# Loading, rounding and subtracting the first four chunks' first matrices by blocks of channels

## The chip, the cores and the metric

The kernel runs on one core of one Trainium2 chip. The metric is the device time of one execution in microseconds (us). Engines are named as in the profile: PE is TensorE (PEld its weight loads), DVE is VectorE, ACT is ScalarE, POOL is GpSimd, SP is SyncE, whose queue issues nearly all DMAs.

## What is computed

The reference, cut to what matters:

```python
# attention: batch 2, 8 heads, 576 positions, head size 64, window of 64 keys
scores = q @ k.T / 8, masked to 0 <= i - j < 64
attn = softmax(scores);  x = attn @ v            # -> x: 1152 tokens x 512
# four experts, all of them on every token
p = domain_probs / domain_probs.sum(-1)
out = sum over e of p[:, e] * (relu(x @ w1[e]) @ w2[e])      # 512 -> 1024 -> 512
# last network
h = out @ w_in;  result = (h * cos(h)) @ w_out   # 512 -> 2048 -> 512
```

Every large product is made of three matmuls in a reduced format: both operands are split into a rounded part (`_hi`) and what rounding left (`_lo`), and hi x hi, hi x lo and lo x hi are added up.

## The kernel before

**Tiling.** The 1152 tokens are three tiles of 384. The attention is cut into 12 units m = 0 to 11, one for each tile and each pair of heads; a unit fills one of the four channel blocks (128 channels each) of x for its tile. Units 0 to 3 (`AHEAD` = 4) give tile 0. The hidden layer of an expert is cut into 8 chunks f of 128 hidden units; a chunk's weights are 128 partitions x 1024 numbers: the first 512 (the chunk's first matrix, for x @ w1) are four blocks of 128 columns, one for each channel block c of x, and the other 512 are the second matrix (for the product with w2).

**Staging of weights.** A chunk comes by DMA into `w_raw` (four slots). ACT or DVE rounds it into `w_hi`. POOL subtracts, `w_lo` = `w_raw` - `w_hi`, in pieces of 256 numbers (L424). Of expert 0's first four chunks (`FIRST` = 4) the two matrices are handled apart: `load_half(f, 0)` loads the first matrix of chunk f (L317), `high_half(f)` rounds it (ACT L589 for f = 0, 1; DVE L846 for f = 2, 3), `low_half(f)` subtracts (L428). `load_half(f, 1)`, `high_second(f)` and `low_second(f)` (L435) do the same for the second matrix. Chunk 4 comes whole into a spare buffer inside `h_raw` (L341) and is treated by `high_ahead` and `low_ahead` (L598, L439). Chunks 5, 6 and 7 are loaded by `load_later` (L321) into slots 0, 1, 2 of `w_raw`: it waits until `low_second(slot)` has read the slot for the last time.

**The attention of a unit.** PE `scores(m)` (L1109); DVE `masked_maxima(m, h)` (L816) for both heads h; ACT `exponentials(m, h)` (L568); DVE `invert_sums(m, h)` (L829); POOL `normalise(m, h)` (L447, the line of its instruction is L450); PE `transpose_probs(m, h)` (L1127, instruction L1142); DVE copies of the transposed rows, `copy_first` (L836) and `copy_second_early` (L841), from unit 4 on ACT `copy_second` (L579); PE `outputs(m)` (L1145); ACT `x_high(m)` (L585); DVE `x_low(m)` (L850).

**The first product runs under the attention.** As soon as unit m has filled channel block m of x, PE runs `up_ahead(m, fs)` (L1170): the products of block m for the chunks fs, three matmuls (L1166) for each chunk. So c = 0 uses only the first block of 128 columns of each first matrix, c = 1 the second one, and so on. Only for c = 0 does `up_ahead` wait for weights, chunk by chunk (L1173, L1174).

**Order.** Each engine's order is written out by hand. PE's is at L1352 to L1415, POOL's at L455 to L481, ACT's at L720 to L763, DVE's at L1010 to L1069, SP's at L327 to L362. Each engine and each queue works strictly in its written order; a wait at one instruction holds all that stands behind it.

Of the kernel before, what the change touches and what calls it, by code (L numbers as in the profile page):

```python
# [108 lines left out]
def build(nc, q, k, v, probs, weights, out):  # L109
    with ExitStack() as ctx:  # L110
# [3 lines left out]
        def sem(name):  # L114
            return ctx.enter_context(nc.semaphore(name))
# [98 lines left out]
        x_hi_done = sem("x_hi_done")  # L214
        x_lo_done = sem("x_lo_done")
        dp_in, dp_done, p_picked = sem("dp_in"), sem("dp_done"), sem("p_picked")
        half_in = [sem(f"half_in{i}") for i in range(FIRST)]
        w_in_done = [sem(f"w_in_done{i}") for i in range(STAGE)]
        second_in = [sem(f"second_in{i}") for i in range(FIRST)]
        ahead_in = sem("ahead_in")  # L220
        half_hi_done = sem("half_hi_done")
        half_hi_done_dve = sem("half_hi_done_dve")
        half_lo_done = sem("half_lo_done")
        second_hi_done = sem("second_hi_done")
        second_lo_done = sem("second_lo_done")
        w_hi_done = sem("w_hi_done")
# [68 lines left out]
        def _(sp):  # L295
            def load_qk(m):
                t, c, r = m // PAIRS, m % PAIRS, m % SLOTS
                if m >= SLOTS:
                    sp.wait_ge(scored, m - SLOTS + 1)
                sp.dma_start(q_t[:, r, :], q[c, :, t * TOK:(t + 1) * TOK]).then_inc(q_in[r], 16)  # L300
                n = TOK if t == 0 else KEYS
                sp.dma_start(k_t[:, r, 0:n], k[c, :, KEY0[t]:KEY0[t] + n]).then_inc(k_in[r], 16)

            def load_v(m):
                t, c, r = m // PAIRS, m % PAIRS, m % SLOTS
                if m >= SLOTS:
# [7 lines left out]
                sp.wait_ge(w_lo_done, n - STAGE + 1)  # L314
                sp.dma_start(w_raw[:, f % STAGE, :], weights[e, f]).then_inc(w_in_done[f % STAGE], 16)

            def load_half(f, half, landed):  # L317
                cols = slice(half * DM, (half + 1) * DM)
                sp.dma_start(w_raw[:, f, cols], weights[0, f, :, cols]).then_inc(landed[f], 16)

            def load_later(f):  # L321

                slot = f - FIRST - 1
                sp.wait_ge(second_lo_done, slot + 1)
                sp.dma_start(w_raw[:, slot, :], weights[0, f]).then_inc(w_in_done[slot], 16)

# [2 lines left out]
            load_qk(1)  # L329
            load_qk(2)  # L330
            load_v(0)
            for f in range(FIRST):
                load_half(f, 0, half_in)
            load_qk(3)
            load_v(1)
            load_qk(4)
            load_v(2)
            load_half(0, 1, second_in)
            load_qk(5)
            load_v(3)  # L340
            sp.dma_start(w_ahead, weights[0, FIRST]).then_inc(ahead_in, 16)  # L341
            load_half(1, 1, second_in)
            load_qk(6)
            load_half(2, 1, second_in)
            load_v(4)
            load_later(5)
            load_half(3, 1, second_in)
            load_qk(7)
            load_v(5)
            load_qk(8)  # L350
# [7 lines left out]
            load_qk(11)  # L358
            for e in range(1, E):
                load_v(8 + e)  # L360
            sp.wait_ge(second_lo_done, FIRST)
            sp.wait_ge(w_lo_done, FC)  # L362
            def load_block(e, f):
# [24 lines left out]
        def _(pool):  # L388
# [32 lines left out]
            def low_part(f, raw, begin, end, part):  # L421

                for at in range(begin, end, part):
                    last = nc.gpsimd.tensor_tensor(w_lo[:, f, at:at + part], raw[:, at - begin:at - begin + part],  # L424
                                                   w_hi[:, f, at:at + part], ALU.subtract)
                return last

            def low_half(f):  # L428
                if f < FIRST // 2:
                    pool.wait_ge(half_hi_done, f + 1)  # L430
                else:
                    pool.wait_ge(half_hi_done_dve, f - FIRST // 2 + 1)
                low_part(f, w_raw[:, f, 0:DM], 0, DM, PART).then_inc(half_lo_done, 1)

            def low_second(f):  # L435
                pool.wait_ge(second_hi_done, f + 1)
                low_part(f, w_raw[:, f, DM:2 * DM], DM, 2 * DM, PART).then_inc(second_lo_done, 1)
# [18 lines left out]
            normalise(0, 1)  # L456
            nc.gpsimd.memset(half_pi[:, :], 0.0).then_inc(half_pi_zeroed, 1)
            normalise(1, 0)
            low_half(0)
            normalise(1, 1)  # L460
            low_half(1)
            low_half(2)
            low_half(3)
            normalise(2, 0)
            normalise(2, 1)
            normalise(3, 0)
            low_second(0)
            normalise(3, 1)
            normalise(4, 0)
            low_ahead(FIRST, w_ahead)  # L470
            normalise(4, 1)
# [89 lines left out]
        def _(act):  # L561
# [24 lines left out]
                act.wait_ge(attended, m + 1)  # L586
                nc.scalar.activation(x_hi[x_cell(m)], o_bank(m)[:, 0:TOK], ACT.Copy).then_inc(x_hi_done, 1)

            def high_half(f):  # L589
                act.wait_ge(half_in[f], 16)  # L590
                nc.scalar.activation(w_hi[:, f, 0:DM], w_raw[:, f, 0:DM], ACT.Copy).then_inc(half_hi_done, 1)

            def high_second(f):
                act.wait_ge(second_in[f], 16)
# [125 lines left out]
            exponentials(0, 0)  # L720
            exponentials(0, 1)
            exponentials(1, 0)
            high_half(0)
            exponentials(1, 1)
            high_half(1)
            for m in range(AHEAD):
                if m > 0:
                    exponentials(m + 2, 0)
# [71 lines left out]
        def _(dve):  # L800
# [42 lines left out]
                nc.vector.tensor_copy(prob_t[:, 1, :, :], pt_bank(m, 1)[:, 0:TOK].rearrange(  # L843
                    "p (t c) -> p t c", t=CT)).then_inc(second_copied_early, 1)

            def high_half(f):  # L846
                dve.wait_ge(half_in[f], 16)
                nc.vector.tensor_copy(w_hi[:, f, 0:DM], w_raw[:, f, 0:DM]).then_inc(half_hi_done_dve, 1)
# [173 lines left out]
            copy_second_early(0)  # L1022
            masked_maxima(2, 1)
            invert_sums(1, 1)
            high_half(2)
            x_low(0)
            high_half(3)
            copy_first(1)
            copy_second_early(1)
            masked_maxima(3, 0)  # L1030
# [4 lines left out]
            for m in range(2, AHEAD):  # L1035
                invert_sums(m + 1, 0)
                masked_maxima(m + 2, 0)
                copy_first(m)
                masked_maxima(m + 2, 1)
                copy_second_early(m)  # L1040
                invert_sums(m + 1, 1)
                x_low(m)
            masked_maxima(AHEAD + 2, 0)
            masked_maxima(AHEAD + 2, 1)
# [59 lines left out]
        def _(pe):  # L1104
# [64 lines left out]

            def up_ahead(c, fs):  # L1170

                for f in fs:
                    if c == 0:  # L1173
                        pe.wait_ge(half_lo_done, f + 1)  # L1174
                    last = up_cells(y_ps[f], f, 0, (c,))
                    if c == DC - 1:
                        last.then_inc(up_done, 1)
# [301 lines left out]
```

## Time and profile before

| | us |
|---|---|
| median of 3 runs | 640.38 (640.38 to 641.29) |
| profiled execution, its own time | 639.62 |
| its span in the trace | 637.7 |
| PE busy | 629.2 (99% of the span) |
| DVE, ACT, POOL busy | 305.2, 260.3, 272.2 |

The 1.92 us between span and own time lie around the program. The profile page gives the busy time of each engine, the chain of work that ended last, and the costliest groups of instructions; a query of the trace gives the instructions in order of time, with the idle time in front of each and the one that ended it. Times in the trace count from the span's start.

### The profile page before, as it was taken

The page shows a single profiled execution, that of the slowest core. Times are in us where ns is not written, and L with a number is a line of the kernel's source. Part 1 is how long each engine was busy: PE and PEld are TensorE (multiplying, and loading weights), DVE is VectorE, ACT ScalarE, POOL GpSimd, SP SyncE. Part 2 cuts the span into 40 slices and gives each one's busy share as a digit, 9 for nine tenths or more (in the row PEclk, how much of TensorE's full clock was granted, in tenths as well). Part 3 has the DMA queues.
Part 4 walks back from the last instruction along what each step waited for, and adds up shares of the span by engine and source line. Part 5 has one row for each costly group of instructions (what it writes and reads, how often), then busy time and mean ns, then how long its engine had stood idle before and what let it go on. Part 6 is the DMA issues. An engine that isn't in the chain of part 4 may idle for free.

```text
span 637.7 us, 10145 instructions
## 1 busy us (share of the span) xinstructions
PE 629.2 (99%) x3656; PEld 561.9 (88%) x3656; DVE 305.2 (48%) x722; ACT 260.3 (41%) x554; POOL 272.2 (43%) x404
## 2 busy tenths in 40 slices
PE   7999999999999999999999999999999999999998
PEld 5887899999989998989998888989999999999996
DVE  6754431215433315433315433426775666766564
ACT  6776322233321223321223321246655467544542
POOL 6783246698720296720296720287000059400000
PEclk9999999999999999999999999999999999999999
DMA  9874100022120011220012120033100012001011
GB/s 285 273 226 151 44 1 1 1 56 77 67 66 1 1 66 66 66 66 0 1 66 67 67 66 1 26 107 100 34 0 1 1 38 96 1 0 49 0 51 50
DMA packets 21896, 37.25 MB, mean 58 GB/s; under 512 B 2784, under 2 KB 14048, under 8 KB 21856
## 3 DMA queue, kind: packets, MB, share of 16 engines
q1 hardware_dynamic: 20688, 36.71, 17.7%
q8 instruction: 24, 0.39, 0.2%
q10 hardware_dynamic: 1168, 0.02, 0.1%
q14 instruction: 16, 0.13, 0.1%
HBM read 34.36 MB, written 2.36 MB: 58 GB/s over the span
## 4 chain that ended last, share of the span: by engine, by line
PE 96%; DVE 1%; POOL 1%; ACT 1%; issue 0%; DVEq 0%
PE bank L1166 31%; PE bank L1194 31%; PE bank L1225 16%; PE bank L1211 14%; PE bank L1158 2%; PE bank L1122 1%; PE bank L1142 1%; PE bank L1308 1%; DVE s_sb L823 1%; PE bank L1350 1%; POOL w_lo L424 0%; ACT prob L574 0%; DVE acc L973 0%; POOL prob L450 0%; DVE prob_t L838 0%
## 5 line engine op out<-in xcount | busy, mean ns | idle before, releaser
L424 POOL TENSOR_TENSOR w_lo<-w_raw,w_hi 128x128 fp32r<-128x128 f32 (+1 forms) x252 | 150.6, 633 | 214.4 <-ACT w_hi L606 211.9
L1166 PE MATMUL bank<-x_hi,w_hi 128*128 128x384 f32 (+1 forms) x384 | 131.2, 342 | 0.5 <-POOL w_lo L424 0.5
L1166 PE MATMUL bank<-x_hi,w_lo 128*128 128x384 f32 (+1 forms) x384 | 129.1, 336 | 0.0
L1166 PE MATMUL bank<-x_lo,w_hi 128*128 128x384 f32 (+1 forms) x384 | 128.7, 335 | 0.0
L1194 PE MATMUL bank<-w_hi,hp_hi 128*128 128x512 f32 x288 | 114.7, 398 | 0.1
L1194 PE MATMUL bank<-w_hi,hp_lo 128*128 128x512 f32 x288 | 113.4, 394 | 0.0
L1194 PE MATMUL bank<-w_lo,hp_hi 128*128 128x512 f32 x288 | 112.1, 389 | 0.0
L926 DVE TENSOR_TENSOR h_raw<-bank,h_raw 128x384 f32<-128x384 f32 x84 | 46.6, 555 | 91.9 <-PE bank L1211 91.9
L1166 PEld LDWEIGHTS bank<-x_hi,w_hi 128*128 128x128 f32 x384 | 72.1, 188 | 3.6 <-POOL w_lo L424 0.8
L1166 PEld LDWEIGHTS bank<-x_lo,w_hi 128*128 128x128 f32 x384 | 72.2, 188 | 1.5
L857 DVE SCALAR_TENSOR_TENSOR hp_lo<-bank,hp_hi 128x384 fp32r<-128x384 f32 x48 | 26.5, 556 | 98.1 <-ACT hp_hi L638 57.5
L1166 PEld LDWEIGHTS bank<-x_hi,w_lo 128*128 128x128 f32 x384 | 72.1, 188 | 0.0
L1194 PEld LDWEIGHTS bank<-w_lo,hp_hi 128*128 128x128 f32 x288 | 54.1, 188 | 12.2
L630 ACT ACTIVATE hp_hi<-h_raw 128x384 fp32r<-128x384 f32 x48 | 25.3, 528 | 94.2 <-DVE h_raw L926 94.2
L1194 PEld LDWEIGHTS bank<-w_hi,hp_hi 128*128 128x128 f32 x288 | 54.0, 188 | 10.9 <-issue 0.4
L1194 PEld LDWEIGHTS bank<-w_hi,hp_lo 128*128 128x128 f32 x288 | 54.2, 188 | 8.5
L1225 PE MATMUL bank<-w_hi,hp_hi 128*128 128x512 f32 x144 | 56.6, 393 | 0.0
L1225 PE MATMUL bank<-w_hi,hp_lo 128*128 128x512 f32 x144 | 56.5, 392 | 0.0
L1225 PE MATMUL bank<-w_lo,hp_hi 128*128 128x512 f32 x144 | 56.1, 390 | 0.0
L606 ACT ACTIVATE w_hi<-w_raw 128x1024 fp32r<-128x1024 f32 x40 | 42.1, 1052 | 11.7 <-PE bank L1194 11.7
L992 DVE TENSOR_TENSOR h_raw<-c_cos,bank 128x384 f32<-128x384 f32 x48 | 26.6, 554 | 37.1 <-ACT c_cos L701 37.1
L699 ACT ACTIVATE c_abs<-c_r 128x384 f32<-128x384 f32 x48 | 25.3, 527 | 42.5 <-DVE c_r L984 42.4
(103 smaller groups left out, 966.4 us busy)
## 6 DMA issues: line engine op xcount, KB each, us to landing
w_raw<-in_weights SPq DMA_DIRECT2D x43, 512.0 KB, 3.7
q_t<-in_q SPq DMA_DIRECT2D x12, 192.0 KB, 4.3
result<-acc SPq DMA_DIRECT2D x9, 256.0 KB, 2.0
w_raw<-in_weights SPq DMA_DIRECT2D x8, 256.0 KB, 5.8
k_t<-in_k SPq DMA_DIRECT2D x8, 224.0 KB, 5.3
v_w<-in_v SPq DMA_DIRECT2D x4, 384.0 KB, 5.0
v_w<-in_v SPq DMA_DIRECT2D x4, 320.0 KB, 6.5
k_t<-in_k SPq DMA_DIRECT2D x4, 192.0 KB, 3.7
```

The costliest lines, as they stand in the source:

```text
L424: last = nc.gpsimd.tensor_tensor(w_lo[:, f, at:at + part], raw[:, at - begin:at - begin + part], w_hi[:, f, at:at + part], ALU.subtract)
L606: nc.scalar.activation(w_hi[:, f, :], w_raw[:, f % STAGE, :], ACT.Copy).then_inc(w_hi_done, 1)
L630: nc.scalar.activation(hp_hi[:, i, :], h_raw[:, i, :], ACT.Relu).then_inc(pair_hi_done, 1)
L699: nc.scalar.activation(c_abs, c_r2, ACT.Abs).then_inc(cos_abs, 1)
L857: nc.vector.scalar_tensor_tensor(out=hp_lo[:, f % HP, :], in0=ps[:, 0:TOK], scalar=0.0, in1=hp_hi[:, f % HP, :], op0=ALU.max, op1=ALU.subt ...
L926: nc.vector.tensor_tensor(h_raw[:, place, :], ps, h_raw[:, other, :], ALU.add).then_inc(pair_taken, 1)
L992: nc.vector.tensor_tensor(h_raw[:, f % HP, :], c_cos, bank_h, ALU.mult).then_inc(cos_taken, 1)
L1158: last = nc.tensor.matmul(o_bank(m)[heads, block_of * WIN:(block_of + 1) * WIN], v_w[:, r, WINDOW_OF[t][block_of], heads], prob_t[:, h, bl ...
L1166: last = nc.tensor.matmul(ps[:, 0:TOK], w[:, f, chunk(c)], x[:, c, token_cols(t)], start=c == 0 and i == 0, stop=c == DC - 1 and i == 2)
L1194: last = nc.tensor.matmul(y_ps[c][:, :], h[:, f % HP, chunk(c)], w[:, f, DM:2 * DM], start=f == 0 and i == 0, stop=f == FC - 1 and i == 2)
L1211: last = nc.tensor.matmul(bank[(g * PRODUCTS + j) % 2][:, 0:TOK], a, b, start=c == 0 and i == 0, stop=c == 1 and i == 2)
L1225: last = nc.tensor.matmul(pair_y[t][c][:, :], h[:, i, chunk(c)], w[:, f, DM:2 * DM], start=f == 0 and k == 0, stop=f == FC - 1 and k == 2)
```

## The change

The first matrices of chunks 0 to 3 are no longer handled chunk by chunk but block by block. `load_channels(c)` loads channel block c of all four chunks in one DMA of the same 256 KB (runs of 128 numbers, 512 bytes, where a half had runs of 2 KB). `high_channels(c)` rounds it, ACT for c = 0, 1 and DVE for c = 2, 3. `low_channels(c)` subtracts it, as two instructions of 2 x 128 numbers. `up_ahead(c, fs)` waits for block c. The five orders change with it.

```diff
+            def load_channels(c):
+                sp.dma_start(w_raw[:, :, chunk(c)],
+                             weights[0, 0:FIRST, :, chunk(c)].rearrange("f p n -> p f n")).then_inc(channels_in[c], 16)
...
             def load_later(f):
                 slot = f - FIRST - 1
+                sp.wait_ge(channels_lo_done, DC)
                 sp.wait_ge(second_lo_done, slot + 1)
...
-            def low_half(f):
-                if f < FIRST // 2:
-                    pool.wait_ge(half_hi_done, f + 1)
-                else:
-                    pool.wait_ge(half_hi_done_dve, f - FIRST // 2 + 1)
-                low_part(f, w_raw[:, f, 0:DM], 0, DM, PART).then_inc(half_lo_done, 1)
+            def low_channels(c):
+                if c < DC // 2:
+                    pool.wait_ge(channels_hi_done, c + 1)
+                else:
+                    pool.wait_ge(channels_hi_done_dve, c - DC // 2 + 1)
+                for f in range(0, FIRST, 2):
+                    part = (slice(None), slice(f, f + 2), chunk(c))
+                    last = nc.gpsimd.tensor_tensor(w_lo[part], w_raw[part], w_hi[part], ALU.subtract)
+                last.then_inc(channels_lo_done, 1)
...
             normalise(1, 0)
-            low_half(0)
+            low_channels(0)
             normalise(1, 1)
-            low_half(1)
-            low_half(2)
-            low_half(3)
+            low_channels(1)
             normalise(2, 0)
             normalise(2, 1)
+            low_channels(2)
             normalise(3, 0)
+            normalise(3, 1)
+            low_channels(3)
             low_second(0)
-            normalise(3, 1)
             normalise(4, 0)
             low_ahead(FIRST, w_ahead)
...
+            def high_channels(c):
+                dve.wait_ge(channels_in[c], 16)
+                nc.vector.tensor_copy(w_hi[:, 0:FIRST, chunk(c)], w_raw[:, :, chunk(c)]).then_inc(channels_hi_done_dve, 1)
...
             invert_sums(1, 1)
-            high_half(2)
             x_low(0)
-            high_half(3)
             copy_first(1)
...
                 copy_second_early(m)
                 invert_sums(m + 1, 1)
+                high_channels(m)
                 x_low(m)
...
             def up_ahead(c, fs):
+                pe.wait_ge(channels_lo_done, c + 1)
                 for f in fs:
-                    if c == 0:
-                        pe.wait_ge(half_lo_done, f + 1)
```

ACT's two roundings keep their places (`high_channels(0)` and `(1)` where `high_half(0)` and `(1)` stood). PE's instructions keep their order; only their waits change.

**POOL, from `normalise(1, 0)` to `normalise(4, 1)`.** `prob` rows are `normalise`, `w_lo` rows are the subtractions; two pieces make one half, one block or one second matrix. Before:

```order
L450 TENSOR_TENSOR prob<-prob,row_inv 128x384
L424 TENSOR_TENSOR w_lo<-w_raw,w_hi 128x256 x2
L450 TENSOR_TENSOR prob<-prob,row_inv 128x384
L424 TENSOR_TENSOR w_lo<-w_raw,w_hi 128x256 x6
L450 TENSOR_TENSOR prob<-prob,row_inv 128x384 x3
L424 TENSOR_TENSOR w_lo<-w_raw,w_hi 128x256 x2
L450 TENSOR_TENSOR prob<-prob,row_inv 128x384 x2
L424 TENSOR_TENSOR w_lo<-h_raw,w_hi 128x256 x4
L450 TENSOR_TENSOR prob<-prob,row_inv 128x384
```

The same stretch of POOL after the change:

```order
L462 TENSOR_TENSOR prob<-prob,row_inv 128x384
L444 TENSOR_TENSOR w_lo<-w_raw,w_hi 128x2x128 x2
L462 TENSOR_TENSOR prob<-prob,row_inv 128x384
L444 TENSOR_TENSOR w_lo<-w_raw,w_hi 128x2x128 x2
L462 TENSOR_TENSOR prob<-prob,row_inv 128x384 x2
L444 TENSOR_TENSOR w_lo<-w_raw,w_hi 128x2x128 x2
L462 TENSOR_TENSOR prob<-prob,row_inv 128x384 x2
L444 TENSOR_TENSOR w_lo<-w_raw,w_hi 128x2x128 x2
L433 TENSOR_TENSOR w_lo<-w_raw,w_hi 128x256 x2
L462 TENSOR_TENSOR prob<-prob,row_inv 128x384
L433 TENSOR_TENSOR w_lo<-h_raw,w_hi 128x256 x4
L462 TENSOR_TENSOR prob<-prob,row_inv 128x384
```

Blocks 2 and 3 moved from behind `normalise(1, 1)` to in front of `normalise(3, 0)` and in front of `low_second(0)` and `normalise(4, 0)`.

**DVE, at the end of the work for unit 2.** The names: `copy_second_early(2)`, `invert_sums(3, 1)`, `x_low(2)`. Before:

```order
L843 COPY prob_t<-bank 128x384
L832 TENSOR_SCALAR row_inv<-row_sum 128x3
L834 RECIPROCAL row_inv<-row_inv 128x3
L852 TENSOR_TENSOR x_lo<-bank,x_hi 128x384
```

After the change, at the same place:

```order
L856 COPY prob_t<-bank 128x384
L845 TENSOR_SCALAR row_inv<-row_sum 128x3
L847 RECIPROCAL row_inv<-row_inv 128x3
L861 CAST w_hi<-w_raw 128x4x128
L865 TENSOR_TENSOR x_lo<-bank,x_hi 128x384
```

The rounding of block 2 now stands behind the copy of unit 2's second transposition; that of block 3 stands at the same place one unit later. Before, DVE's two roundings stood around `x_low(0)`, two units earlier.

## Rows read from the trace of the kernel before

**Rows 1.** The page: busy us, share of the span and instructions of each engine.

```profile
PE 629.2 (99%) x3656; PEld 561.9 (88%) x3656; DVE 305.2 (48%) x722; ACT 260.3 (41%) x554; POOL 272.2 (43%) x404
```

**Rows 2.** Waits of PE over the span: us in total, times, longest.

```profile
PE bank L1142 <- POOL prob L450: 0.8, 2, 0.6
```

**Rows 3.** Timeline of PE: start, us, what, count, idle before and its releaser.

```profile
14.77 0.34 PE L1166 MATMUL bank<-x_hi,w_lo 128*128 128x384 f32 x1
15.60 0.44 PE L1166 MATMUL bank<-x_hi,w_hi 128*128 128x384 f32 x1 [0.49 <-POOL w_lo L424]
...
20.74 0.49 PE L1142 MATMUL bank<-ident,prob 128*128 128x128 f32 x3
...
23.90 0.55 PE L1142 MATMUL bank<-ident,prob 128*128 128x128 f32 x3
...
25.85 0.52 PE L1142 MATMUL bank<-ident,prob 128*128 128x128 f32 x3 [0.20 <-DVE prob_t L838]
...
29.02 0.55 PE L1142 MATMUL bank<-ident,prob 128*128 128x128 f32 x3
...
31.64 0.49 PE L1142 MATMUL bank<-ident,prob 128*128 128x128 f32 x3
...
34.08 0.39 PE L1194 MATMUL bank<-w_hi,hp_hi 128*128 128x512 f32 x1
```

**Rows 4.** Timeline of POOL, same columns.

```profile
11.60 1.42 POOL L424 TENSOR_TENSOR w_lo<-w_raw,w_hi 128x256 fp32r<-128x256 f32 x2
12.97 1.01 POOL L450 TENSOR_TENSOR prob<-prob,row_inv 128x384 f32<-128x384 f32 x1
13.94 4.37 POOL L424 TENSOR_TENSOR w_lo<-w_raw,w_hi 128x256 fp32r<-128x256 f32 x6
18.28 2.40 POOL L450 TENSOR_TENSOR prob<-prob,row_inv 128x384 f32<-128x384 f32 x3
...
25.87 2.81 POOL L424 TENSOR_TENSOR w_lo<-h_raw,w_hi 128x256 fp32r<-128x256 f32 x4 [0.40 <-ACT w_hi L600]
28.63 0.85 POOL L450 TENSOR_TENSOR prob<-prob,row_inv 128x384 f32<-128x384 f32 x1
```

**Rows 5.** Timeline of DVE, same columns.

```profile
12.48 0.81 DVE L848 CAST w_hi<-w_raw 128x512 fp32r<-128x512 f32 x1
...
13.68 0.58 DVE L848 CAST w_hi<-w_raw 128x512 fp32r<-128x512 f32 x1
...
21.27 0.56 DVE L843 COPY prob_t<-bank 128x384 f32<-128x384 f32 x1 [0.17 <-PE bank L1142]
21.74 0.35 DVE L832 TENSOR_SCALAR row_inv<-row_sum 128x3 f32<-128x3 f32 x1
...
24.20 0.16 DVE L832 TENSOR_SCALAR row_inv<-row_sum 128x3 f32<-128x3 f32 x1
...
24.51 0.29 DVE L823 CUSTOM_DVE_ANT_0 s_sb<-bank,mask 128x128 f32<-128x128 f32 x1
```

**Rows 6.** DMA to landing: first v of unit 3 (issued 12.27), then chunk 5 (22.10).

```profile
DMA to landing us min/median/max: 8.3/8.3/8.3
...
DMA to landing us min/median/max: 4.4/4.4/4.4
```

**Rows 7.** Timeline of ACT, same columns.

```profile
23.20 0.49 ACT L587 ACTIVATE x_hi<-bank 128x384 fp32r<-128x384 f32 x1 [1.89 <-PE bank L1158]
...
30.39 1.05 ACT L600 ACTIVATE w_hi<-w_raw 128x1024 fp32r<-128x1024 f32 x1
31.34 0.47 ACT L676 ACTIVATE hp_hi<-bank 128x384 fp32r<-128x384 f32 x1
```

**Rows 8.** One stretch: us, busy of PE, PEld, DVE, ACT, POOL, PEclk, DMA, GB/s.

```profile
10.00:12.00 2.00, 0.99 (x18) 0.78 (x20) 1.84 (x11) 2.00 (x9) 1.44 (x4) 1.00 1.07 374
```

**Rows 9.** PE's weight loads at L1350, first before 4.5 us, then from 8.

```profile
L1350 PEld LDWEIGHTS bank<-zeros x14: 287/333/333, 1.3 to 4.1; 128*128 128x128 f32 x14
...
L1350 PEld LDWEIGHTS bank<-zeros x6: 186/192/192, 8.2 to 8.8; 128*128 128x128 f32 x6
```

More of the change, by code:

```diff
@@ L216, in build @@
         dp_in, dp_done, p_picked = sem("dp_in"), sem("dp_done"), sem("p_picked")
-        half_in = [sem(f"half_in{i}") for i in range(FIRST)]
+        channels_in = [sem(f"channels_in{i}") for i in range(DC)]
         w_in_done = [sem(f"w_in_done{i}") for i in range(STAGE)]
@@ L220, in build @@
         ahead_in = sem("ahead_in")
-        half_hi_done = sem("half_hi_done")
-        half_hi_done_dve = sem("half_hi_done_dve")
-        half_lo_done = sem("half_lo_done")
+        channels_hi_done = sem("channels_hi_done")
+        channels_hi_done_dve = sem("channels_hi_done_dve")
+        channels_lo_done = sem("channels_lo_done")
         second_hi_done = sem("second_hi_done")
@@ L315, in load_chunk, with load_second @@
                 sp.dma_start(w_raw[:, f % STAGE, :], weights[e, f]).then_inc(w_in_done[f % STAGE], 16)
-            def load_half(f, half, landed):
-                cols = slice(half * DM, (half + 1) * DM)
-                sp.dma_start(w_raw[:, f, cols], weights[0, f, :, cols]).then_inc(landed[f], 16)
+            def load_channels(c):
+                sp.dma_start(w_raw[:, :, chunk(c)],
+                             weights[0, 0:FIRST, :, chunk(c)].rearrange("f p n -> p f n")).then_inc(channels_in[c], 16)
+            def load_second(f):
+                cols = slice(DM, 2 * DM)
+                sp.dma_start(w_raw[:, f, cols], weights[0, f, :, cols]).then_inc(second_in[f], 16)
             def load_later(f):
                 slot = f - FIRST - 1
+                sp.wait_ge(channels_lo_done, DC)
                 sp.wait_ge(second_lo_done, slot + 1)
@@ L331, in _ @@
             load_v(0)
-            for f in range(FIRST):
-                load_half(f, 0, half_in)
+            load_channels(0)
             load_qk(3)
             load_v(1)
+            load_channels(1)
             load_qk(4)
             load_v(2)
-            load_half(0, 1, second_in)
+            load_channels(2)
             load_qk(5)
             load_v(3)
+            load_channels(3)
+            load_second(0)
             sp.dma_start(w_ahead, weights[0, FIRST]).then_inc(ahead_in, 16)
-            load_half(1, 1, second_in)
+            load_second(1)
             load_qk(6)
-            load_half(2, 1, second_in)
+            load_second(2)
             load_v(4)
             load_later(5)
-            load_half(3, 1, second_in)
+            load_second(3)
             load_qk(7)
@@ L360, in _ @@
                 load_v(8 + e)
+            sp.wait_ge(channels_lo_done, DC)
             sp.wait_ge(second_lo_done, FIRST)
@@ L587, in x_high @@
                 nc.scalar.activation(x_hi[x_cell(m)], o_bank(m)[:, 0:TOK], ACT.Copy).then_inc(x_hi_done, 1)
-            def high_half(f):
-                act.wait_ge(half_in[f], 16)
-                nc.scalar.activation(w_hi[:, f, 0:DM], w_raw[:, f, 0:DM], ACT.Copy).then_inc(half_hi_done, 1)
+            def high_channels(c):
+                act.wait_ge(channels_in[c], 16)
+                nc.scalar.activation(w_hi[:, 0:FIRST, chunk(c)], w_raw[:, :, chunk(c)],
+                                     ACT.Copy).then_inc(channels_hi_done, 1)
             def high_second(f):
@@ L722, in _ @@
             exponentials(1, 0)
-            high_half(0)
+            high_channels(0)
             exponentials(1, 1)
-            high_half(1)
+            high_channels(1)
             for m in range(AHEAD):
@@ L844, in copy_second_early, with high_channels @@
                     "p (t c) -> p t c", t=CT)).then_inc(second_copied_early, 1)
-            def high_half(f):
-                dve.wait_ge(half_in[f], 16)
-                nc.vector.tensor_copy(w_hi[:, f, 0:DM], w_raw[:, f, 0:DM]).then_inc(half_hi_done_dve, 1)
+            def high_channels(c):
+                dve.wait_ge(channels_in[c], 16)
+                nc.vector.tensor_copy(w_hi[:, 0:FIRST, chunk(c)], w_raw[:, :, chunk(c)]).then_inc(channels_hi_done_dve, 1)
             def x_low(m):
```

## The prediction

> **What bounds the kernel now.** I read the page first, then the waits of PE, then the four engines' timelines between 11 and 38 us. The page shows PE busy for 629.2 of 637.7 us [rows 1]: whatever the first weights cost or give must show as a wait of PE, and a wait that PE gains or loses there is never made up or taken back later, since the other 600 us are PE's own work. The waits tell where PE is near the edge in the attention part: not at weights as a rule, but at `normalise` on POOL, 0.8 us in two waits [rows 2]. The timeline shows the one wait that the change is about: the second `up_ahead(0)` product starts at 15.60 after 0.49 us of waiting for `low_half(1)` on POOL [rows 3]. POOL is full there: `normalise(1, 1)` and the three halves behind it run without a gap from 12.97 to 18.28 [rows 4]. From 20.68 (18.28 + 2.40) POOL is ahead of PE: `normalise(3, 0)`, the last of the three in that row, is done 3.2 us before PE's transposition of unit 3 asks for it at 23.90 [rows 3, 4]. This lead of POOL is what the change touches.
>
> **What it removes.** `low_channels(0)` serves all four chunks, so PE's wait at 15.60 goes. The matmuls of one product follow one another in 0.17 us, so the product would start at 14.94 (14.77 + 0.17) and PE runs 0.66 us earlier from there [rows 3]. What is late next: `outputs(1)` needs DVE's copy of unit 1, in front of which DVE now has two casts less, so the gain holds. PE would then reach the second transposition of unit 2 at 20.08 instead of 20.74 [rows 3]. DVE loses two casts before `copy_first(1)`; that frees DVE, which PE doesn't wait for there: nothing. The matmuls are the same in number and order: nothing.
>
> **What it moves, first place.** `normalise(3, 0)` now stands behind `low_channels(2)`, which waits for DVE's `high_channels(2)`, which stands behind `copy_second_early(2)`, which waits for PE's second transposition of unit 2. So a chain starts at 20.08 that didn't exist before. Its steps, start to start:
> - transposition to copy 0.53 (20.74 to 21.27) [rows 3, 5];
> - copy 0.47 (21.27 to 21.74) [rows 5];
> - `invert_sums(3, 1)` 0.31 with POOL idle (24.20 to 24.51) [rows 5];
> - the cast of 512 numbers. No cast of four runs of 128 is in the trace. The two casts of one run took 0.73 (12.48 to 13.21) and 0.50 (13.68 to the copy behind it at 14.18), both beside a busy POOL; of the second only 0.24 lies behind POOL's change of instruction at 13.94 [rows 4, 5]. Bounds 0.24 and 0.73; I take 0.50, the undisturbed start and end;
> - `low_channels(2)`, two pieces: 1.42, as for two pieces of 256 [rows 4]. Its 2 x 128 shape isn't in the trace; `normalise`, also a shape of several runs, takes 0.80 for 384 numbers (2.40 for three), so I see no reason for more, and bound it by 1.37 and 1.6;
> - `normalise(3, 0)` 0.80 [rows 4].
>
> Sum 4.03, so the transposition of unit 3 starts at 24.11, against 23.90 before: the whole gain of 0.66 is gone, and 0.21 is lost. Handoffs at POOL are left out; they add some 0.1.
>
> **Between.** The second transposition of unit 3 was at 25.85, held by `copy_first(3)` on DVE, which stood behind `x_low(2)` and so behind ACT's `x_high(2)` at 23.20 [rows 3, 7]. ACT stays near 23.20 (see the loads below). I take 25.80; bounds 25.55 (24.11, a transposition and two products) and 25.95.
>
> **What it moves, second place.** This costs more, since two things stand in front of `normalise(4, 0)` now: `low_channels(3)`, at the end of the same chain one unit later, and behind it `low_second(0)`, which had long been done. From 25.80: 0.53 + 0.47 + 0.31 + 0.50 + 1.42 + 1.42 + 0.80 = 5.45, with the same rows and the same bounds for the cast; `low_second(0)` ends at 30.45 and `normalise(4, 0)` at 31.25. PE's first transposition of unit 4 was at 29.02 [rows 3]: 2.23 late. Then POOL still owes `low_ahead(4)`, 2.76 (25.87 to 28.63), and `normalise(4, 1)`, 0.85 [rows 4], so the second transposition of unit 4 starts at 34.86, not 31.64 [rows 3]. **PE is 3.22 us late there.** Before, `low_ahead(4)` ran under PE's work on unit 3.
>
> **Behind it.** SP's queue stops at `load_later(5)` until `low_second(0)` is done: 30.45, not 22.10. Queued behind it are the second matrix of chunk 3 and the inputs of units 7 and 8, all wanted after 38 us. Chunk 5 landed 4.4 us after its issue [rows 6]; that gives 34.85. ACT's `high_ahead(5)` waits for it (1.05) and in front of it stands ACT for `hidden_high(0)` (0.47) and DVE's low part (about 0.5) [rows 7]: 36.9. PE wants it for the first `down_cells` at 34.08 + 3.22 = 37.30 [rows 3]. So this wait is hidden, by 0.4 us only. POOL's other work keeps its distance to PE, which is now 3.2 us later. The new loads in 512-byte runs: the first block is loaded in the place of the first half; the second has 704 KB of q, k and v in front of it in place of 0, and ACT wants it in front of `x_high(0)`. DVE and PE have to wait for POOL there before they need `x_high(0)`, and DVE has its two casts' time (1.2 us) to make up a delay of it: nothing. `load_second(0)` falls behind the inputs of unit 3, which landed at 20.57 (12.27 + 8.3) [rows 6]; with 0.6 for itself and some for short runs it lands at about 21.4, ACT stops for it, and `x_high(2)` comes at about 23.1: as before [rows 7].
>
> **One rule against one row.** The cast's row of 12.48 shows 0.81 us, and it ends 0.24 behind POOL's change of instruction at 12.97; `invert_sums` took 0.35 beside POOL and 0.16 without it [rows 4, 5]. In the changed kernel POOL is idle during both casts. The Trainium skill ("SBUF — State Buffer", section "SBUF: two separate sides") says that VectorE in a two-port mode and GpSimd take a shared port pair in turn, each for a whole instruction; "VectorE: DVE Perf Modes" (perf-mode tier table) gives fp32 copies in SBUF that mode. The rows agree. By that rule both casts would take some 0.3, an estimate, and the sum would be 0.4 smaller.
>
> **The sum.** The profiled execution of 639.62 (1.92 around its span) would become 642.84, with a span of 640.9. The median of the runs is 640.38, 0.76 higher; 640.38 + 3.22 = **643.6 us**. With both casts at 0.24 and 25.55 in between: -0.77, 642.8. With both at 0.73, pieces at 1.6 and 25.95: +1.2, 644.8.
>
> **The rivals.**
> - *The late load decides* (15%). If chunk 5 lands later than 4.8 us after its issue, or `load_second(0)` after 21.5, ACT holds PE. The input of unit 3 took 8.3 in a full queue [rows 6]; against it, at 30.45 the queue has been empty for microseconds. At 6 us for chunk 5: 34.08 becomes 38.5, 4.4 late, 644.8; with both late 645.5.
> - *PE's clock falls* (12%). PE would stand still for some 2.2 us in front of 31.25 and 1 us in front of 34.86. The granted clock is 1.00 also from 10 to 12 us, where PE is busy for 0.99 of 2 us [rows 8], which speaks against it; on the other hand the first weight loads at L1350 take 333 ns and those after 8 us 192 [rows 9], so the lower level (1.2 GHz against 2.4) may exist here without the column showing it. Two to four microseconds of matmuls at that pace, partly under the wait for POOL, cost 1 to 2: 645.4. The Trainium skill ("TensorE: Matmul & The Clock Gate", "HAM oscillation — how this bites in real kernels") tells of kernels whose clock drops in pauses between bursts; no pause as long is in this trace once PE has started.
> - *Only the gain stays* (4%). PE keeps the 0.66 us and both `normalise` come in time: 639.7. It decides at the first chain: it must take less than 3.8 us (20.08 to 23.90), and the second less than 3.2 (25.85 to 29.02). The first sums to 4.03 and 3.5 at the lowest, so it could; the second to 5.45 and 4.9 at the lowest, with 1.42 + 0.80 in it that no cast can hide. For it speaks only that I may misread an order.
> - *The change doesn't do what it says, or the two ends meet* (6%): the chains overlap better than written and about 1 us is lost, 641.4.
>
> **How the numbers follow.** The forecast (642.8 to 644.8) has 63%, the late load 15%, the clock 12%, only the gain 4%, a small loss 6%. The range 642.7 to 645.6 leaves out the last two and a tail of the first three. 0.2% (1.28 us) is about what a measurement of this kernel can tell from no change; 3.2 us is 0.5%. Slower by over 0.2%: 0.91; within: 0.06; faster: 0.03.
>
> **What would show it.** In the changed profile: no wait of PE for `w_lo` near 15; POOL idle from about 18 to 22 with DVE's `w_hi` as its releaser; PE waiting for `prob` of L462 at about 24.1 (1 us), 31.3 (over 2 us) and 34.9 (about 1 us), 4 us in all against 0.8 [rows 2]; SP's chunk 5 issued near 30.5. I am wrong if POOL has done `normalise(4, 0)` by 29, if PE waits for ACT near 37, or if the rest of the span, from 38 us on, isn't a copy of before.

## The result, and the profile after

| | before | after |
|---|---|---|
| median of 6 runs, us | 640.4 (639.79 to 641.29) | 643.07 (642.89 to 644.8) |
| profiled execution, its own time | 639.62 | 644.44 |
| its span | 637.7 | 642.4 |
| PE busy | 629.2 | 631.6 |

The changed kernel is slower: ratio 1.0049, 95% interval 1.0038 to 1.0059; the medians differ by 2.67 us. Forecast were 643.6 us and a range of 642.7 to 645.6. In some executions PE's granted clock falls for a few microseconds; the profiled one of after is such a one (mean clock 0.995; 4 of its 6 runs took 642.89 to 643.07), so part of its trace has to be read beside that of another execution.

First the waits of PE over the span (us in total, times, longest), against [rows 2]:

```profile
PE bank L1154 <- POOL prob L462: 3.7, 4, 2.2
PE bank L1134 <- DVE neg_max L836: 1.4, 2, 1.0
```

L462 is `normalise`: 3.7 us where it was 0.8. There is no row of PE waiting for `w_lo` any more. PE's timeline (start, us, what, count, idle before and its releaser) answers to [rows 3]. Its rows are the transposition (1,1), the second product of block 0, where the old wait stood, then transpositions (2,1), (3,0), (3,1), (4,0), (4,1), and the first `down_cells`:

```profile
15.46 0.55 PE L1154 MATMUL bank<-ident,prob 128*128 128x128 f32 x3
...
16.37 0.34 PE L1178 MATMUL bank<-x_hi,w_hi 128*128 128x384 f32 x1
...
21.44 0.52 PE L1154 MATMUL bank<-ident,prob 128*128 128x128 f32 x3
...
25.49 0.55 PE L1154 MATMUL bank<-ident,prob 128*128 128x128 f32 x3 [0.80 <-POOL prob L462]
...
26.95 0.52 PE L1154 MATMUL bank<-ident,prob 128*128 128x128 f32 x3
...
32.36 0.74 PE L1154 MATMUL bank<-ident,prob 128*128 128x128 f32 x3 [2.17 <-POOL prob L462]
...
36.42 0.49 PE L1154 MATMUL bank<-ident,prob 128*128 128x128 f32 x3
...
38.86 0.39 PE L1205 MATMUL bank<-w_hi,hp_hi 128*128 128x512 f32 x1
```

POOL's timeline of the same stretch, against [rows 4], shows why. It stands still for 3.31 and 2.53 us, waiting for DVE's roundings, and then owes PE `normalise` behind the subtractions:

```profile
23.23 1.41 POOL L444 TENSOR_TENSOR w_lo<-w_raw,w_hi 128x256 fp32r<-128x256 f32 x2 [3.31 <-DVE w_hi L861]
24.60 1.61 POOL L462 TENSOR_TENSOR prob<-prob,row_inv 128x384 f32<-128x384 f32 x2
28.74 1.41 POOL L444 TENSOR_TENSOR w_lo<-w_raw,w_hi 128x256 fp32r<-128x256 f32 x2 [2.53 <-DVE w_hi L861]
30.11 1.41 POOL L433 TENSOR_TENSOR w_lo<-w_raw,w_hi 128x256 fp32r<-128x256 f32 x2
31.47 0.83 POOL L462 TENSOR_TENSOR prob<-prob,row_inv 128x384 f32<-128x384 f32 x1
32.26 2.79 POOL L433 TENSOR_TENSOR w_lo<-h_raw,w_hi 128x256 fp32r<-128x256 f32 x4
35.00 0.84 POOL L462 TENSOR_TENSOR prob<-prob,row_inv 128x384 f32<-128x384 f32 x1
```

DVE's timeline, against [rows 5], has the other half of the chain for unit 2: copy, inversion, rounding.

```profile
22.00 0.56 DVE L856 COPY prob_t<-bank 128x384 f32<-128x384 f32 x1
22.47 0.16 DVE L845 TENSOR_SCALAR row_inv<-row_sum 128x3 f32<-128x3 f32 x1
...
22.76 0.40 DVE L861 CAST w_hi<-w_raw 128x512 fp32r<-128x512 f32 x1
```

Read the three together from 21.44: copy at 22.00, inversion 22.47, rounding 22.76, subtraction 23.23, `normalise(3, 0)` 24.60, transposition 25.49. Each step starts when the one before ends, and between the two transpositions all of them lie on other engines.

What this execution has beside the chains is the clock. One stretch per microsecond (us, busy of PE, PEld, DVE, ACT, POOL, PEclk, DMA, GB/s):

```profile
11.00:12.00 1.00, 0.26 (x6) 0.19 (x7) 0.87 (x5) 1.00 (x7) 0.91 (x2) 1.00 1.08 345
12.00:13.00 1.00, 1.00 (x24) 1.00 (x22) 0.81 (x6) 0.59 (x2) 1.00 (x2) 0.55 1.14 327
13.00:14.00 1.00, 1.00 (x11) 0.55 (x8) 0.23 (x1) 0.76 (x3) 1.00 (x2) 0.50 1.21 295
...
31.00:32.00 1.00, 0.00 (x0) 0.00 (x0) 0.77 (x8) 0.58 (x2) 1.00 (x2) 1.00 0.00 0
...
33.00:34.00 1.00, 1.00 (x5) 1.00 (x5) 0.56 (x1) 0.00 (x0) 1.00 (x2) 0.50 0.81 274
```

PE is granted half its clock from 12 to about 15.5 us, after a pause (0.74 us in front of `outputs(0)`), and again from 32.4 to 35.8, after it had stood still for 2.17. The first fall costs 1.3 us: from `outputs(0)` at 11.84 to transposition (1,1) at 15.46 are 3.62 us, against 2.30 in an execution at full clock (12.23 to 14.53, experiment 4, filled at 10 and 11). The pause alone doesn't bring the fall about: in the 2 us in front of `outputs(0)` PE was busy for 0.72 here and for 0.71 in the profiled execution of before, whose clock stayed at 1.00.

### The profile page after: what moved, and what is told of

It is laid out like the page before. It is cut to its first block, busy times and chain, and to the rows that moved or that the text cites. A ratio compares the mean times of both kernels' runs of the same rounds, so it can differ in the third digit from the quotient of the medians.

```text
span 642.4 us, 10151 instructions
## 1 busy us (share of the span) xinstructions
PE 631.6 (98%) x3656; PEld 564.9 (88%) x3656; DVE 304.3 (47%) x722; ACT 259.6 (40%) x554; POOL 271.7 (42%) x404
## 4 chain that ended last, share of the span: by engine, by line
PE 96%; DVE 1%; POOL 1%; ACT 0%; issue 0%; DVEq 0%
PE bank L1178 31%; PE bank L1205 31%; PE bank L1236 15%; PE bank L1222 14%; PE bank L1170 1%; PE bank L1154 1%; PE bank L1134 1%; PE bank L1319 1%; PE bank L1361 1%; DVE s_sb L836 0%; POOL w_lo L444 0%; POOL prob L462 0%; ACT prob L586 0%; DVE acc L986 0%; DVE prob_t L856 0%
## 5 line engine op out<-in xcount | busy, mean ns | idle before, releaser
L433 POOL TENSOR_TENSOR w_lo<-w_raw,w_hi 128x128 fp32r<-128x128 f32 (+1 forms) x244 | 144.8, 629 | 212.8 <-ACT w_hi L619 211.8
```

## Experiments

All kernels are edits of the changed one. "Base" is after's code. (m,h) is head h of unit m. Medians of before from the same chip and hour stand beside each, since the two must be compared there.

**1. Both roundings moved forward on DVE.** The whole theory is that `high_channels(2)` and `(3)` stand too far back on DVE.

```diff
             invert_sums(2, 1)
+            high_channels(2)
             x_low(1)
...
                 masked_maxima(m + 2, 1)
+                if m == 2:
+                    high_channels(3)
                 copy_second_early(m)
                 invert_sums(m + 1, 1)
-                high_channels(m)
```

> The changed kernel with DVE's two casts of blocks 2 and 3 moved forward: block 2 in front of x_low(1), block 3 in front of copy_second_early(2). POOL's, ACT's, SP's and PE's orders stay. My theory (the loss is the wait of normalise(3, 0) and normalise(4, 0) for the late casts): both chains are gone, POOL is ahead of PE again, no wait of PE for normalise after 15 us, and the 0.66 us won at 15.6 stays: 639.7. Rival 1 (the later loads, now held until low_second(0) and low_channels(3) are done, set the end through ACT): ACT waits for chunk 5 and PE is late at the first down_cells: 642 to 643. Rival 2 (the new order of POOL costs by its amount of work, wherever the casts are): about 642.4.

Measured: 640.05 us (11 runs), before 640.7 (22 runs), ratio 0.9991 [0.9982, 1.0]. PE's waits in its trace:

```profile
PE bank L1156 <- POOL prob L462: 0.8, 2, 0.5
PE bank L1156 <- DVE prob_t L851: 0.7, 2, 0.6
```

All of the loss goes with two lines' places; blocks, loads and subtractions are as in after. Both waits for `normalise` that are left lie before 12 us. A new one comes: (3,1) waits 0.58 us for `copy_first(3)` (experiment 7). A gain over before isn't shown: the interval reaches 1.0, and from (1,1) to the first `down_cells` the traces have 19.90 us here and 20.05 before. Part of the 0.65 between the medians is the clock: 10 of before's 22 executions had a mean clock of 0.997, 2 of these 11.

**2. Only block 3's rounding moved forward**, right behind block 2's (it can't come before it without a change of semaphores).

```diff
                 invert_sums(m + 1, 1)
-                high_channels(m)
+                if m == 2:
+                    high_channels(2)
+                    high_channels(3)
```

> The changed kernel with DVE's cast of block 3 alone moved forward, right behind that of block 2 (behind copy_second_early(2)). My theory: the first chain stays (transposition of unit 3 waits 0.8 us for POOL), the second one goes; but low_channels(3) and low_second(0) then run from 25.6 to 28.4 without a pause, normalise(4, 0) comes at about 29.2 just in time, and low_ahead(4) and normalise(4, 1) end at 32.9, 1.2 us behind the time of before: 641.6. Rival 1 (late loads): chunk 5 is issued 2.6 us earlier than in the changed kernel, 640.5. Rival 2 (clock): PE no longer stands still for 2.2 us, no fall near 32 us; that alone would give 642.6.

Measured: 640.83 us (11 runs), ratio to before 1.0007 [0.9998, 1.0017]. Without the second chain the loss against before is no longer told from nothing; against experiment 1, with the same before beside it, 0.78 us are left for the first chain. From (1,1) to the first `down_cells` are 20.55 us, against 22.97 with both chains (the clean column below) and 19.90 with neither. PE's timeline shows the first chain alone, what is left at (4,1), and a wait that neither before nor after has, for a copy on DVE behind 38 us:

```profile
24.68 0.55 PE L1156 MATMUL bank<-ident,prob 128*128 128x128 f32 x3 [0.93 <-POOL prob L462]
...
32.59 0.55 PE L1156 MATMUL bank<-ident,prob 128*128 128x128 f32 x3 [0.49 <-POOL prob L462]
...
42.36 0.52 PE L1156 MATMUL bank<-ident,prob 128*128 128x128 f32 x3 [0.48 <-DVE prob_t L851]
```

The expectation was 0.8 too high: it put `normalise(4, 1)` 1.2 us behind PE, and PE waits 0.49 for it. POOL works without a pause from 22.30 on and is done with it at 32.54, where 32.9 was expected, and PE's (1,1) lies 0.49 later here than in the trace of before that the expectation counted from.

**3. `low_second(0)` in front of `low_channels(2)` on POOL**, to take 1.42 us out of the second chain.

```diff
             normalise(2, 1)
+            low_second(0)
             low_channels(2)
...
             low_channels(3)
-            low_second(0)
```

> The changed kernel with low_second(0) moved in front of low_channels(2), where POOL stands idle for 3.3 us; nothing else moves. My theory: the second chain is shorter by this one piece of work, 1.37 us, so normalise(4, 0) and all behind it come 1.37 us earlier and the time falls by as much, from 643.07 to 641.7. Rival 1 (late loads): load_later(5) still waits for low_channels(3), its issue moves from 31.6 to 30.1 at best, 641.6 too, but then with PE waiting for ACT in front of the first down_cells. Rival 2 (clock): PE's pause shrinks to 0.8 us and the fall near 32 us goes; 0.5 more, 641.2.

Measured: 642.93 us (6 runs), ratio 1.0034 [1.0022, 1.0046], where 641.7 was expected: 0.14 less than after by the medians. ACT's timeline, then POOL's and PE's tell why:

```profile
20.85 0.64 ACT L608 ACTIVATE w_hi<-w_raw 128x512 fp32r<-128x512 f32 x1 [1.65 <-DMA w_raw<-in_weights]
```

```profile
21.57 1.60 POOL L433 TENSOR_TENSOR w_lo<-w_raw,w_hi 128x256 fp32r<-128x256 f32 x2 [2.58 <-ACT w_hi L608]
23.13 1.41 POOL L444 TENSOR_TENSOR w_lo<-w_raw,w_hi 128x256 fp32r<-128x256 f32 x2
```

```profile
25.38 0.55 PE L1154 MATMUL bank<-ident,prob 128*128 128x128 f32 x3 [1.65 <-POOL prob L462]
...
30.84 0.55 PE L1154 MATMUL bank<-ident,prob 128*128 128x128 f32 x3 [0.81 <-POOL prob L462]
```

The 1.4 us did leave the second chain (2.19 to 0.81 us of waiting at (4,0)), but `low_second(0)` waited there for ACT, whose operand is loaded late, and pushed the first chain back by 0.84 (0.81 to 1.65). I had taken it for ready; its own load says otherwise. Of the 0.60 us that are left of the gain at the first `down_cells` (22.37 from (1,1), against 22.97), 0.28 go to a wait for a copy on DVE at 43.88, as in experiment 2.

**4. Does the clock count?** Idle 128-column matmuls on zeros (their result isn't read) keep PE busy in its pauses: six in front of (4,0) in `e4_fill_wait`, four in all near 10 and 11.3 us in `e5_fill_early`, both in `e8_both_fills`.

```diff
+                    pe.wait_ge(x_lo_done, AHEAD)
+                    keep_busy(6, bank[0])        # e4, e8: in front of transposition (4,0)
...
             transpose_probs(0, 0)
+            keep_busy(2, y_ps[2])                # e5, e8
             transpose_probs(0, 1)
+            keep_busy(2, y_ps[2])
             outputs(0)
```

> The changed kernel with six idle matmuls of zeros (into a free bank) in PE's pause in front of the first transposition of unit 4, behind a wait for x_low(3). My theory: POOL sets the time there, PE's work after the pause is hidden by low_ahead(4) also at half clock but for 0.5 us (36.42 against 35.84 for the end of normalise(4, 1)); so the granted clock near 32 to 36 stays at 1.00 or falls less, and the time moves by 0 to -0.5 us: 642.6 to 643.1. Rival 2 (the clock carries a good part of the loss): 641.5 or less.

> The changed kernel with two idle matmuls of zeros (into a free bank) in each of PE's two first pauses, in front of the second transposition of unit 0 and in front of outputs(0) (0.54 and 0.74 us of waiting). The profile of the changed kernel shows the granted clock at 0.5 from 12 to 15.5 us, other executions of before and after have a mean clock of 0.997 and take 0.5 to 1 us more than those at 1.00. If PE's pauses between 9 and 12 us let the clock fall, no execution does so here: all runs near 643.0, none at 644 or over. If the pauses have nothing to do with it, a third of the runs is at 644 or over as before. The chains at POOL, and so the median of the changed kernel, stay.

> As the one with the early idle matmuls, and the six idle matmuls in front of the first transposition of unit 4 too. It differs from that one only in the clock from 32 to 36 us. My theory (POOL sets the time there): 0 to 0.5 us less than that one. Rival 2 (the clock carries a good part of the loss): 1 us or more less.

| | us | ratio to before |
|---|---|---|
| filled at 30 | 644.21 (642.34 to 644.44, 5 runs) | 1.005 [1.0037, 1.0064] |
| filled at 10 and 11 | 642.95 (642.78 to 647.07, 6 runs) | 1.0055 [1.0035, 1.0075] |
| both | 643.21 (642.99 to 643.88, 5 runs) | 1.0048 [1.0035, 1.0061] |

Neither place makes the kernel faster: all three intervals overlap that of after (1.0049). The first expectation (642.6 to 643.1) is missed by its median, the last one (0 to 0.5 less than with the early filling alone) by 0.26, which is within the spread of the runs; its profiled execution (643.79) stands still for 0.50 us at 18.82, for which the profile names no releaser.

The mean clocks of the single runs say more. A fall of about 3.5 us shows as a mean clock of 0.997, two of them as 0.995. After's two runs at 0.995 took 644.44 and 644.8; its two at 0.997 (642.89, 643.07) took no longer than its two at 1.00 (643.07). Filled at 30, three of five runs have 0.997 and took 644.21 to 644.44, so the fall that is left there costs over 1 us. Filled early, three of six have 0.997: two took 642.83 and 643.05, as those at 1.00, and the third took 647.07, which contradicts what was expected, and I have no trace of it. With both places filled none of five has it. This reads as one early fall that costs over 1 us and one late fall that costs nearly nothing, but only after's own trace shows where they lie. Where the long pause is gone and the early ones are filled (experiments 6 and 7), none of 33 runs is at 0.997; of before's 69 runs beside the experiments 24 are, and their medians lie 0.5 to 1 us above those of the others. The clock adds a tail, it is not the 2.7 us.

The profiled execution with the early filling runs at full clock all through, and so gives the clean reading of the chains. PE's timeline of it, from (1,1) on:

```profile
14.53 0.55 PE L1154 MATMUL bank<-ident,prob 128*128 128x128 f32 x3
...
20.52 0.52 PE L1154 MATMUL bank<-ident,prob 128*128 128x128 f32 x3
...
24.57 0.55 PE L1154 MATMUL bank<-ident,prob 128*128 128x128 f32 x3 [0.81 <-POOL prob L462]
...
26.04 0.52 PE L1154 MATMUL bank<-ident,prob 128*128 128x128 f32 x3
...
31.46 0.55 PE L1154 MATMUL bank<-ident,prob 128*128 128x128 f32 x3 [2.19 <-POOL prob L462]
...
35.03 0.55 PE L1154 MATMUL bank<-ident,prob 128*128 128x128 f32 x3 [0.92 <-POOL prob L462]
...
37.50 0.39 PE L1205 MATMUL bank<-w_hi,hp_hi 128*128 128x512 f32 x1
```

**5. The loads alone.** The weights come as four halves in 2 KB runs, one after the other in the first place, as before, and are still rounded and subtracted by blocks. Each rounding waits for all four loads, and the other three block loads go, so the later loads move forward: `load_second(0)` takes the place of `load_channels(2)`.

```diff
-            load_channels(0)
+            for f in range(FIRST):
+                load_half(f)
...
-            load_channels(2)
+            load_second(0)
```

> The changed kernel with the weights of blocks loaded as before: four loads of one chunk's first matrix each, in runs of 2 KB, early in the queue; each rounding waits for all four. Rounding, subtracting, and the orders of ACT, DVE, POOL and PE are those of the change. My theory (the loads are hidden, only order costs): the time of the changed kernel, 643.0. Rival 1 (later and finer loads cost): ACT's wait of 0.35 us for the second matrix of chunk 0 goes and the time falls by 0.5 or more.

Measured: 644.21 us (643.59 to 645.05, 5 runs), ratio 1.0064 [1.0051, 1.0077], where 643.0 was expected: slower than after by 1.1 by the medians, though the intervals overlap, and by 0.5 in the traces at full clock (643.59 against 643.06). ACT's timeline:

```profile
11.58 0.63 ACT L601 ACTIVATE w_hi<-w_raw 128x512 fp32r<-128x512 f32 x1 [0.86 <-DMA w_raw<-in_weights]
```

Block 0 needs 256 KB; by halves it needs all 1 MB, and (1,1) comes 0.38 us later (14.91 against 14.53). The rival that made the later and finer loads a cost falls, since without them nothing is gained. What the short runs cost by themselves the experiment can't tell, as it changes the waits with them.

**6. Roundings early and pauses filled** (experiments 1 and 4 together), a first try for a version that beats both.

> DVE's casts of both blocks early, and the early idle matmuls: meant to beat both kernels. With my theory, 0.66 us less than before in runs at full clock and no runs at a lower mean clock: 639.5 to 640.0, and a narrower spread than the kernel with the casts alone (639.4 to 641.2).

Measured: 639.97 us (639.42 to 640.39, 11 runs), before 640.32, ratio 0.9995 [0.9986, 1.0004]. The narrowest spread of the kernels with 11 runs so far and no run at a mean clock below 0.999, as expected, but not told apart from before: PE's wait at 15.6 is gone, and the new one at (3,1) takes 0.58 us back (experiment 7).

**7. The next wait.** In experiments 1 and 6 (3,1) waits for `copy_first(3)`:

```profile
26.18 0.52 PE L1156 MATMUL bank<-ident,prob 128*128 128x128 f32 x3 [0.58 <-DVE prob_t L851]
```

Moved forward on DVE is first that copy (`e9_copy_sooner`), then `copy_second_early(3)` too (`e10_both_copies`). DVE's order behind `x_low(2)`, for m = 3:

```diff
+                copy_first(3)
                 invert_sums(4, 0)
                 masked_maxima(5, 0)
-                copy_first(3)
+                copy_second_early(3)         # only e10_both_copies
                 masked_maxima(5, 1)
-                copy_second_early(3)         # only e10_both_copies
                 invert_sums(4, 1)
```

> All of the changed kernel, with both DVE casts early and PE's pauses at 10 and 11 us filled, and one more move on DVE: copy_first(3) stands in front of invert_sums(4, 0) and masked_maxima(5, 0) instead of behind them. In the trace without this move PE waits 0.58 us at the second transposition of unit 3 (26.18) for copy_first(3) at 25.48, while DVE does 1.3 us of other work from 24.15 on; with it the copy can start when x_low(2) ends, near 24.7, and the wait goes. Theory (PE's waits are all that counts, nothing else is near the edge): 0.58 less than the same kernel without the move, 640.0 - 0.6 = 639.4, with before at 640.3, a ratio of 0.9986. POOL's normalise(4, 0) ended 2.5 us before PE wanted it and may come 0.5 later. Rival (another wait takes its place, the next in line being ACT's x_high(3) or POOL's normalise(4, 1), done 1.6 us before it is wanted): 640.0, no change against the kernel without the move.

> The kernel with both casts early, the pauses filled and copy_first(3) moved forward, with one more move: copy_second_early(3) stands in front of masked_maxima(5, 1) instead of behind it. In the trace without this move the waits of PE for DVE at the second transposition of unit 3 are gone, but outputs(3) waits 0.47 us (26.89) for copy_second_early(3), which starts at 26.23 behind masked_maxima(5, 1), 0.84 us of DVE's work, although the transposition it copies has ended at 25.36. Theory: with the move the copy starts at 25.4 and the 0.47 goes; 639.5 - 0.5 = 639.0 against 640.3 of before, a ratio of 0.998. Rival (what PE gains here it waits for at normalise(4, 1) or at ACT's work on unit 3, so nothing more comes out): 639.5. normalise(4, 1) ends at 29.8 and is wanted at 31.2 without the move, so it should hold 1.4 us of further gain.

Measured: 639.46 us (11 runs), ratio 0.9987 [0.9977, 0.9996], and 639.36 (638.62 to 639.77, 11 runs), ratio 0.9984 [0.9975, 0.9993], before 640.31 both times. With the first move alone a wait takes the place of the one removed, in front of `outputs(3)`. PE's row, and the copy on DVE that `outputs(3)` needs:

```profile
26.89 0.92 PE L1175 MATMUL bank<-prob_t,v_w 128*64 128x64 f32 x24 [0.47 <-issue]
```

```profile
26.23 0.55 DVE L856 COPY prob_t<-bank 128x384 f32<-128x384 f32 x1
```

The row names no releaser; that it is the copy is read from its end at 26.78 and from the second move, behind which the wait is gone.

With both, PE runs from 12.2 us on without a wait of 0.2 us or more up to the first `down_cells`, and the last rows of its timeline read:

```profile
25.47 0.49 PE L1161 MATMUL bank<-ident,prob 128*128 128x128 f32 x3
...
28.61 0.55 PE L1161 MATMUL bank<-ident,prob 128*128 128x128 f32 x3
...
31.24 0.49 PE L1161 MATMUL bank<-ident,prob 128*128 128x128 f32 x3
...
33.67 0.39 PE L1212 MATMUL bank<-w_hi,hp_hi 128*128 128x512 f32 x1
```

From the same start ((3,0) at 23.87 here, 23.86 in experiment 6) the first `down_cells` comes 0.7 us earlier (33.67 against 34.40); the medians give 0.6. The median of this version is 0.95 us below that of before and 3.7 below that of after. Against before not all of it is the order: 7 of the 15 executions of before in that hour had a mean clock of 0.997, the other 8 a median of 639.72. From (1,1) to `down_cells`, at full clock in both traces, are 19.16 us here and 20.05 before. The second move was expected to give 0.5 us. From (3,0) to `down_cells` the traces have 10.34 us with the first move and 9.80 with both, but the step between the medians (639.46 and 639.36) is smaller than these measurements tell apart.

## Why the prediction was right, and where it was off

Between transposition (1,1) and the first `down_cells` the stretch falls into the prediction's own steps. The clean column is the execution at full clock (experiment 4, filled early). In before's trace the stretch starts here:

```profile
14.03 0.55 PE L1142 MATMUL bank<-ident,prob 128*128 128x128 f32 x3 [0.27 <-POOL prob L450]
```

| step | before | predicted | clean | after, profiled |
|---|---|---|---|---|
| (1,1) to (2,1): the removed wait | 6.71 | 6.05 | 5.99 | 5.98 |
| (2,1) to (3,0): first chain | 3.16 | 4.03 | 4.05 | 4.05 |
| (3,0) to (3,1): between | 1.95 | 1.69 | 1.47 | 1.46 |
| (3,1) to (4,0): second chain | 3.17 | 5.45 | 5.42 | 5.41 |
| (4,0) to (4,1): `low_ahead`, `normalise` | 2.62 | 3.61 | 3.57 | 4.06 |
| (4,1) to `down_cells` | 2.44 | 2.44 | 2.47 | 2.44 |
| sum | 20.05 | 23.27 | 22.97 | 23.40 |

- **What was removed.** PE's wait for `low_half(1)` went, and the stretch is 0.72 us shorter, 0.66 predicted.
- **First chain.** 4.05 for 4.03, at the place and with the releaser predicted. The match hides small errors that cancel: the rounding starts 0.47 before the subtraction behind it, not 0.50, the two pieces take 1.37 and not 1.42, and the handoffs left out give 0.1 back (24.60 to 25.49 is 0.89 where `normalise` alone was put at 0.80). Experiment 1, which takes only the chains away, takes the loss away. Where the prediction weighs "only the gain stays", its lowest sums, 3.5 and 4.9, don't come out of its own bounds: a rounding of 0.24 and pieces of 1.37 give 3.72 and 5.09. The conclusions there stand with these too.
- **Between.** 0.22 too long. The step that failed is "held by `copy_first(3)`": with (3,0) late by the first chain, the copy (26.25 to 26.72) was done before PE asked at 26.95. The value was the prediction's own lower bound (25.55 - 24.11 = 1.44).
- **Second chain and its tail.** 5.41 for 5.45 and 3.57 for 3.61. Both of POOL's debts, `low_channels(3)` with `low_second(0)`, and `low_ahead(4)`, cost what was written. In the profiled execution the tail has 0.5 more: POOL's `normalise(4, 1)` is done at 35.84, but PE, at half its clock, comes to it at 36.42. In the clean execution POOL is the later one. Experiment 3 took `low_second(0)` out of this chain, and the wait at (4,0) fell by 1.38; experiment 2 took its wait for the rounding away, and (3,1) to (4,0) is back at 3.17.
- **The late load** stayed hidden. ACT waits 3.56 us for chunk 5, which landed 3.5 us after its issue (4.4 assumed), and PE asks for the result later. `load_second(0)` was put at 21.4; ACT waited for it until 20.49, and `x_high(2)` came as early behind (2,1) as before (2.48 us, 2.46 before).

```profile
35.15 1.06 ACT L613 ACTIVATE w_hi<-w_raw 128x1024 fp32r<-128x1024 f32 x1 [3.56 <-DMA w_raw<-in_weights]
```

- **The loads in short runs** were put at nothing, and PE never waits for a weight. Experiment 5 shows that whole halves in that place would have cost 0.5 to 1.1 us, since the first block would have waited for all four.
- **The clock** rival was right that the clock can fall in such pauses, and wrong about the price: behind the pause at 30 the fall costs 0.5 us (4.06 against 3.57), since POOL is nearly as late, and two executions with pauses of 2.19 and 2.31 us there (experiments 4 and 5) stayed at 1.00. The fall that costs over 1 us lies at 12, behind a pause that before has too. It makes single executions longer, by 1.4 to 1.7 us with both falls, and doesn't move after's median.
- **The rounding's price.** The prediction named the Trainium skill, "SBUF — State Buffer", section "SBUF: two separate sides", by whose rule each rounding would take some 0.3 with POOL idle, the sum being 0.4 smaller. Measured with POOL idle: 0.40. With POOL busy, in the kernel of experiment 6, whose POOL works on `normalise` from 17.37 to 19.13, the same rounding took 1.00, as DVE's timeline shows:

```profile
17.48 1.00 DVE L861 CAST w_hi<-w_raw 128x512 fp32r<-128x512 f32 x1
```

So the trace agrees with the rule's direction: POOL idle or busy makes 0.6 us of difference. The estimate was too low by 0.1, and on the chain the rule was worth 0.03 and not 0.2 for each rounding, since from the start of the rounding to that of the subtraction 0.47 us pass where the sum had 0.50.

**The whole.** The clean stretch is 2.92 us longer than before's, the medians differ by 2.67. The rest lies ahead of (1,1), which kernels with the same code up to there reach up to 0.67 us apart (13.84 in experiment 4, filled at 30, and 14.51 in experiment 3). What decides this no run shows. Of the 0.5 us between 643.6 and 643.07, 0.30 is in the table, 0.22 of it "between"; the rest is this one.

## What to carry to other kernels

Finer pieces of preparation pay only where each piece is also started early: here the same subtractions cost 2.7 us or nothing, by the place of two roundings. When an instruction is moved behind a copy that waits for PE, and something PE needs next is queued behind it, write the whole loop as a chain from PE back to PE and compare it with PE's own work in between; here this gave 4.03 and 5.45 us against 3.16 and 3.17 of cover, and the trace 4.05 and 5.41. Before an instruction is pulled forward in a queue, look at its own input: experiment 3 lost 0.84 of the 1.4 us it gained by one operand that came late. And compare single executions of like clock before medians are compared: part of what looked like a gain over before was executions of before with a fallen clock.

## What the hardware showed unexpectedly

- The granted clock fell to half at 12 us in one execution and stayed there for 3.5 us; 24 score matmuls took 1.56 instead of 0.89 us. The other profiled executions stayed at 1.00 there, with four idle matmuls in the pauses (5 of them) and without (6), and with the same busy time in the 2 us in front (0.71 to 0.72 us without the idle matmuls).
- An fp32 rounding of 128x512 on DVE took 0.40 us beside an idle POOL and, beside a busy one, 0.54 to 1.00.
- A DMA of 256 KB in runs of 512 bytes landed 4.7 us after its issue in the place where the first half was loaded before, and PE never waited for it.
